# One expert of eight in split form: three reduced-precision products in place of full-precision matrix products, in an attention and mixture-of-experts kernel

## The chip, the cores and the metric

The kernel runs on one core of one Trainium2 chip. A core has engines that run side by side, each through its own list of instructions in order, and that wait for each other through semaphores: TensorE (PE, matrix products, its weight loads shown apart as PEld), VectorE (DVE), ScalarE (ACT), GpSimd (POOL) and SyncE (SP, which starts transfers). The metric is the device time of one execution, in microseconds (us); lower is better.

## What is computed

Three layers follow each other, in float32. Only the second and the third matter here.

```python
# layer 1: attention over a window and block summaries, x is 1536 tokens x 512
# layer 2: every token goes to one of E = 8 experts, cap = 192 tokens each
order = np.argsort(-flat)              # greedy: best logits first, experts fill up
...
for e in range(E):
    mask = assigned == e
    h = np.maximum(x[mask] @ w1[e], 0.0)      # 192x512 @ 512x1024
    out[mask] = h @ w2[e]                     # 192x1024 @ 1024x512
# layer 3: dense, on all tokens
h = x @ w_in                                  # 512 -> 1024
sm = e / (np.sum(e, axis=-1, keepdims=True) + 1e-09)   # e = exp(h - max)
solu = h * sm
ln = (solu - mu) / np.sqrt(var + 1e-06) * g_ln
return ln @ w_out                             # 1024 -> 512
```

## The kernel before

The attention runs first. Then come eight rounds, `for r in range(E)`, one expert each, in the order in which experts fill. A round multiplies its 192 tokens by w1 (`hidden`, 8 column blocks `f` by 4 blocks `c` of the depth) and by w2 (`product`, 4 blocks `d` by 8 blocks `c`): 32 and 32 matmuls with 128x128 weights and 192 moving columns, in plain float32. The profile shows each such matmul as two records, so 64 and 64 per round. The dense layer takes tiles of 128 tokens: one after an even round, two after an odd one (12 in all). `dense_in(n)` is the product with w_in and `dense_out(n)` that with w_out. These two are already in split form: each operand is a high part rounded to the type fp32r and a rest (`yT_hi`, `yT_lo`, `win_hi`, `win_lo`, ...), and three products hi*hi, hi*lo, lo*hi are added up in PSUM, 512 columns each. After round r = 6 comes tile 9 (`dense_in(9)`, `dense_out(8)`, in the middle of which the tokens of round 7 are transposed), after round r = 7 tiles 10 and 11.

What goes from PE to the other engines for reuse passes through two PSUM banks, `turn[u % 2]`, as numbered units u: PE fills one and raises `unit_filled`, ACT copies it to SBUF and raises `unit_emptied`, and `unit_free(u)` makes PE wait until unit u - 2 is emptied. A unit of `hidden` or `product` holds two blocks of 192 columns. For `product`, ACT writes `yT_hi` and DVE then writes the rest, `yT_lo` (`split_y`).

Every engine's order is written out by hand. Around the last expert ACT does, for round 6: the relus of `hidden`, the two copies of `yT_hi`, then for tile 9 `empty_turned(8)`, `hidden_exp(9)`, `empty_tokens(7)`, `empty_out(8)`, `hidden_squares(9)`; then the relus of round 7. DVE does `split_y(6, 0)`, `split_y(6, 1)`, `hidden_max(9)`, `split_turned(8)`, `hidden_gate(9)`, `hidden_spread(9)` (which needs the squares), then `split_y(7, 0)`. Weights come by indirect transfers that POOL starts (`gather_w1`, `gather_w2`) into the half `r % 2` of `w1_sb` and `w2_sb`, as soon as the expert two rounds earlier has been multiplied.

Of the kernel before, what the change touches and what calls it, by code (L numbers as in the profile page):

```python
# [5 lines left out]
ALU = mybir.AluOpType  # L6
ACT = mybir.ActivationFunctionType
AX = mybir.AxisListType
# [5 lines left out]
P = 128  # L14
# [49 lines left out]
ROUNDS = E - 1  # L64
PAIRS = E // 2
ROWS = PAIRS * TILES
MASK = -1e9
# [66 lines left out]


def unit_order():
    turned = 2
    for r in range(E):
        yield ("tokens", r), 2
        yield ("hidden", r), FC // 2  # L140
# [17 lines left out]
def build(nc, qT, kT, k_win, vT, v_main, v_tail, w_gate, w1, w2, w_in, w_out, g_ln, consts, digits, x_dram, out):  # L158
    with ExitStack() as ctx:
# [47 lines left out]
        vmean = sb("vmean", [P, D])  # L207

        key_wide = sb("key_wide", [P, NT * P])
        keys = sb("keys", [P, N])  # L210
        neg = keys[:, 0:4 * COLS].rearrange("p (s h c) -> p s h c", s=2, h=2)
# [5 lines left out]
        rden = sb("rden", [P, 2, 2])  # L217
        probT = key_wide[:, 0:6 * P].rearrange("p (s a c) -> p s a c", s=2, a=3)
        xs = sb("xs", [P, LOOP_UN, P])
        wg_sb = sb("wg_sb", [P, 2 * KC, E])  # L220
        xTg = key_wide[:, 6 * P:(6 + GATED) * P].rearrange("p (a c) -> p a c", a=GATED)
# [40 lines left out]


        w1_sb = sb("w1_sb", [P, 2, KC * FF])
        w2_sb = sb("w2_sb", [P, 2, FC * DM])

        kwin = [w[:, 1, 0:QT * SCOLS].rearrange("p (t c) -> p t c", t=QT) for w in (w1_sb, w2_sb)]
# [101 lines left out]
        in_x = [[sem(f"in_x{i}_{part}") for part in ("hi", "lo")] for i in range(2)]  # L369
        h_filled = sem("h_filled")  # L370
        hneg_ready = sem("hneg_ready")
        expo_ready = sem("expo_ready")
# [23 lines left out]
        at = unit_table()  # L396
        y_filled = [at["y", r, 1] + 1 for r in range(E)]
        turned_at = [at["norm", n] + 2 for n in range(ROWS)]
        y_unit = {at["y", r, d]: KC // 2 * r + d + 1 for r in range(E) for d in range(KC // 2)}
        norm_unit = {at["norm", n] + c: 2 * n + c + 1 for n in range(ROWS) for c in range(2)}  # L400

# [314 lines left out]
        def _(act):  # L716
# [72 lines left out]
            def empty_tokens(r):  # L789
# [4 lines left out]
                empty(u, xT[:, :, lo:lo + LO], turn[u % 2][:, 0:KC * LO].rearrange("p (c n) -> p c n", c=KC))  # L794

            def empty_hidden(r, f):
# [37 lines left out]
            for r in range(E):  # L834
                for f in range(FC // 2):
                    empty_hidden(r, f)
                for d in range(KC // 2):
                    empty_y(r, d)
                    if r != 1 and turns_keys(r, 2 * d + 1):
                        empty_keys(r + 2)  # L840
                if r == 1:
                    empty_keys(3, range(2))
                    hidden_exp(0)
                    empty_keys(3, range(2, KEY_UNITS))
                if r == 0:
                    empty_tokens(1)
                for n in tiles_after(r):
                    if n >= 1:
                        empty_turned(n - 1)
                        if n == 1:  # L850
                            hidden_squares(0)
                        hidden_exp(n)
                    if r and n == tiles_after(r)[-1] and r + 1 < E:
                        empty_tokens(r + 1)
# [10 lines left out]
        def _(pe):  # L865
# [127 lines left out]
            def unit_free(u):  # L993
                if u >= 2:
                    pe.wait_ge(unit_emptied, u - 1)
                if u - 2 in y_unit:
                    pe.wait_ge(y_lo_ready, y_unit[u - 2])
                if u - 2 in norm_unit:
                    pe.wait_ge(turned_lo_ready, norm_unit[u - 2])
# [69 lines left out]
            def product(r, d):  # L1069
# [14 lines left out]
                if d % 2:  # L1084
                    mm.then_inc(unit_filled, 1)

            def turn_unit(n, c):

# [9 lines left out]
            def dense_in(n):  # L1098
# [4 lines left out]
                for half in range(2):  # L1103
# [19 lines left out]
                    if half == 0 and j < 2:  # L1123
                        pe.wait_ge(y_lo_ready, 2 * (r + 1))
                    for c in range(KC):
# [39 lines left out]
            def rows_of_round(r):  # L1165
                if r < ROUNDS:
                    row_numbers(r)

            def warm(count):

# [19 lines left out]
            for r in range(E):  # L1190
# [20 lines left out]
                product(r, 3)  # L1211
                if r == 1:
# [29 lines left out]
        def _(dve):  # L1242
# [264 lines left out]
            def split_y(r, d):  # L1507
# [6 lines left out]
                                  yT_hi[part_of].bitcast(F32), ALU.subtract).then_inc(y_lo_ready, 1)  # L1514

            def split_turned(n):
                for c in range(2):
# [155 lines left out]
            for r in (E - 2, E - 1):  # L1673
                split_y(r, 0)
                split_y(r, 1)
                for n in tiles_after(r):
                    hidden_max(n)
                    split_turned(n - 1)
                    hidden_gate(n)
                    hidden_spread(n)  # L1680
            split_turned(ROWS - 1)
            link(dve.tensor_scalar(key_wide[:, N // 2:N].bitcast(BF16), hits, 0.5, 0.0, ALU.is_ge, ALU.add,
                                   accum_out=count[:, :]))
            link(dve.tensor_scalar(hits, keys[:, :], const("cand0"), None, ALU.is_ge))

# [88 lines left out]
```

## Time and profile before

| | |
|---|---|
| median of 3 runs | 498.69 us (498.5 to 498.85) |
| the profiled execution: its own time | 498.7 us |
| its span, first to last instruction | 496.9 us |
| busy: PE, DVE, ACT, POOL | 475.6, 343.5, 169.3, 137.4 us |
| mean granted TensorE clock | 0.993 |

The profiled execution is 1.8 us longer than its span (what lies around it). A time such as 435.24 below is in us from the span's start. Records of matmuls overlap: the time that one takes on the path is the distance from start to start, not its duration.

### The profile page before, as it was taken

The numbers are of one execution on the slowest core, as the hardware profiler recorded it, in microseconds if no ns is written. First come the engines' busy times: TensorE is split into PE (matmuls) and PEld (weight loads), VectorE is DVE, ScalarE is ACT, GpSimd is POOL, SyncE is SP. The second block draws the span as 40 slices with busy tenths as digits, with TensorE's granted clock in tenths as the row PEclk, the third lists the DMA queues.
The fourth block names the chain that finished last, engine by engine and source line by source line (L and its number), as shares of the span: only waits on it lengthen the run. The fifth ranks groups of instructions, "written<-read, shape, count | busy, mean of one in ns | idle before, by whom it ended". The sixth has DMA issues, their size and how long they took to land.

```text
span 496.9 us, 8519 instructions
## 1 busy us (share of the span) xinstructions
PE 475.6 (96%) x2907; PEld 412.5 (83%) x2907; DVE 343.5 (69%) x1180; ACT 169.3 (34%) x436; POOL 137.4 (28%) x206
## 2 busy tenths in 40 slices
PE   7999999989989999999999999999999999999992
PEld 4777777778779889788989988998997899899871
DVE  5777777569889898999869779986975610400451
ACT  3778888830021211343213123322312330320340
POOL 5886667520130130061131014113103231010101
PEclk9999999999999999999999999999999999999997
DMA  8877774110081460064243046034204528000001
GB/s 268 309 248 248 239 237 141 33 34 1 5 325 41 153 218 1 2 222 170 104 173 139 0 170 221 14 126 171 107 0 192 200 87 307 0 22 1 0 22 42
DMA packets 24920, 62.02 MB, mean 125 GB/s; under 512 B 6576, under 2 KB 13616, under 8 KB 20784
## 3 DMA queue, kind: packets, MB, share of 16 engines
q0 software_dynamic: 6592, 39.85, 22.0%
q1 hardware_dynamic: 17280, 20.44, 12.6%
q10 hardware_dynamic: 1008, 1.22, 0.8%
q8 instruction: 23, 0.38, 0.3%
q14 instruction: 17, 0.14, 0.1%
HBM read 55.21 MB, written 6.29 MB: 124 GB/s over the span
## 4 chain that ended last, share of the span: by engine, by line
PE 79%; DVE 13%; DMA 2%; issue 2%; ACT 1%; SPq 1%; POOL 0%; ACTq 0%; DVEq 0%; POOLq 0%
PE psum L1065 15%; PE psum L1082 13%; PE psum L883 6%; DVE key_wide L1406 5%; PE psum L1147 5%; PE psum L1154 5%; PE psum L1148 4%; PE psum L1116 4%; PE psum L1117 4%; PE psum L1126 4%; PE psum L912 4%; PE psum L892 3%; PE psum L909 2%; PE psum L1094 2%; DMA shared<-kT 2%
## 5 line engine op out<-in xcount | busy, mean ns | idle before, releaser
L1406 DVE TENSOR_SCALAR_CACHE_REDUCE key_wide<-keys,thr 128x1536 bf16<-128x1536 f32 x49 | 88.7, 1809 | 1.1
L1082 PE MATMUL psum<-xs,w_sb 128*128 128x192 f32 x512 | 87.0, 328 | 0.0
L1065 PE MATMUL psum<-shared,w_sb 128*128 128x192 f32 x512 | 84.6, 326 | 0.0
L1065 PEld LDWEIGHTS psum<-shared,w_sb 128*128 128x128 f32 x512 | 83.5, 190 | 1.1 <-issue 0.6
L1082 PEld LDWEIGHTS psum<-xs,w_sb 128*128 128x128 f32 x512 | 83.0, 190 | 0.0
L656 POOL DMA_INDIRECT w_sb<-w,widx x32 | 31.3, 979 | 95.4 <-DVE widx L1486 87.6
L680 POOL TENSOR_TENSOR gain<-spread,cst 128x1 f32<-128x1 f32 x12 | 6.8, 567 | 163.3 <-DVE spread L1546 163.3
L1285 DVE CUSTOM_DVE_ANT_0 keys<-psum,w_sb 128x184 f32<-128x184 f32 x96 | 29.7, 347 | 22.6 <-PE psum L883 14.2
L883 PE MATMUL psum<-w_sb,shared 128*128 128x376 f32 x96 | 43.1, 534 | 1.9 <-POOL w_sb L545 1.7
L1513 DVE TENSOR_TENSOR yT_lo<-psum,yT_hi 128x384 fp32r<-128x384 f32 x16 | 8.8, 554 | 51.7 <-ACT yT_hi L779 51.4
L741 ACT ACTIVATE keys<-keys,nmax 128x184 f32<-128x184 f32 x96 | 42.0, 440 | 7.0 <-DVE nmax L1285 6.9
L1147 PE MATMUL psum<-wout_hi,turned_hi 128*128 128x512 f32 x96 | 38.5, 401 | 0.7 <-ACT turned_hi L779 0.7
L1116 PE MATMUL psum<-win_hi,yT_hi 128*128 128x512 f32 x96 | 38.5, 401 | 0.0
L1148 PE MATMUL psum<-wout_lo,turned_hi 128*128 128x512 f32 x96 | 37.6, 391 | 0.0
L1117 PE MATMUL psum<-win_lo,yT_hi 128*128 128x512 f32 x96 | 37.5, 391 | 0.0
L779 ACT ACTIVATE xs<-psum 128x384 f32<-128x384 f32 x32 | 15.6, 489 | 59.0 <-PE psum L1065 59.0
L779 ACT ACTIVATE yT_hi<-psum 128x384 fp32r<-128x384 f32 x16 | 7.9, 491 | 79.5 <-PE psum L1082 79.5
L1172 PE MATMUL psum<-cst 128*128 128x256 f32 x150 | 34.5, 382 | 0.0
L892 PEld LDWEIGHTS psum<-cst,keys 128*128 128x128 f32 x144 | 19.1, 144 | 14.6 <-issue 8.8
L1172 PEld LDWEIGHTS psum<-cst 128*128 128x128 f32 x150 | 27.7, 189 | 3.8
L779 ACT ACTIVATE turned_hi<-psum 128x512 fp32r<-128x512 f32 x24 | 14.1, 597 | 48.2 <-PE psum L1094 48.2
L1126 PE MATMUL psum<-win_hi,yT_lo 128*128 128x512 f32 x96 | 28.6, 402 | 0.0
(176 smaller groups left out, 839.8 us busy)
## 6 DMA issues: line engine op xcount, KB each, us to landing
shared<-vT SPq DMA_DIRECT2D x8, 384.0 KB, 6.0
shared<-v_main SPq DMA_DIRECT2D x8, 384.0 KB, 3.1
x_rows<-xs SPq DMA_DIRECT2D x8, 384.0 KB, 4.8
shared<-kT SPq DMA_DIRECT2D x7, 384.0 KB, 5.5
shared<-qT SPq DMA_DIRECT2D x7, 384.0 KB, 4.9
w_sb<-w_in SPq DMA_DIRECT2D x4, 512.0 KB, 5.4
w_sb<-w_out SPq DMA_DIRECT2D x8, 256.0 KB, 4.6
shared<-v_tail SPq DMA_DIRECT2D x16, 48.0 KB, 3.1
```

What stands on the lines that cost most here:

```text
L741: act.activation(prob[:, s, HEAD1 * hh:HEAD1 * hh + COLS], neg[:, s, hh, :], ACT.Exp, bias=nmax[:, s, hh:hh + 1], scale=-1.0, accum_out=de ...
L779: return act.activation(dst, src, func).then_inc(unit_emptied, 1)
L883: pe.matmul(score[s][:, 0:SCOLS], q_sb[:, b, t * P:(t + 1) * P], kwin[b][:, t, :], start=True, stop=True).then_inc(scores_ready, 1)
L1065: mm = pe.matmul(turn[u % 2][:, i * CAP:(i + 1) * CAP], w1_sb[:, par, first:first + P], xT[:, c, :], start=(c == 0), stop=(c == KC - 1))
L1082: mm = pe.matmul(turn[u % 2][:, (d % 2) * CAP:(d % 2 + 1) * CAP], w2_sb[:, par, first:first + P], hT[:, c, :], start=(c == 0), stop=(c == ...
L1116: pe.matmul(out_cols, yT_hi[:, c, tile], win_hi[:, c, cols], start=(c == 0), stop=False)
L1117: pe.matmul(out_cols, yT_hi[:, c, tile], win_lo[:, c, cols], start=False, stop=False)
L1126: mm = pe.matmul(out_cols, yT_lo[:, c, tile], win_hi[:, c, cols], start=False, stop=(c == KC - 1))
L1147: pe.matmul(pv[:, :], turned_hi[:, c, :], wout_hi[:, c, :], start=(c == 0), stop=False)
L1148: pe.matmul(pv[:, :], turned_hi[:, c, :], wout_lo[:, c, :], start=False, stop=False)
L1172: pe.matmul(pv[:, 0:2 * P], ones_f, slots_f, start=True, stop=True)
L1406: link(dve.tensor_scalar(hits, keys[:, :], cand, -float(CAP), ALU.is_ge, ALU.add, accum_out=count[:, :]))
```

## The change

The last expert, r = 7, is computed in split form. `w1` and `w2` of that expert are rounded by ACT to high parts (four pieces of 128x1024 each), and DVE subtracts these from the raw weights for the rests, in place. The halves of `w1_sb` and `w2_sb` that expert 6 leaves free take the high parts (`w1_split`, `w2_split` lie at the same addresses), so the rounding of w1 waits for the end of `hidden` of round 6, and that of w2 for the end of its `product`. The tokens and the hidden values are kept as pairs (high, rest) side by side, 384 columns. PE multiplies the high weights by the pair (384 columns) and the rest of the weights by the high operand (192 columns), into two halves of a bank; so a unit is now one block `f` or `d`. DVE adds the two halves up (`add_pair`), ACT rounds the sum (relu or copy), and DVE writes the rest. Two DVE instructions at the very end, whose outputs nobody reads, are gone.

```diff
+SPLIT = (E - 1,)
+PIECES = 4
...
+            def round_w2(r, pieces):
+                act.wait_ge(in_w2[r % 2], 32 * (r // 2 + 1))
+                act.wait_ge(unit_filled, y_filled[r - 1])
+                for j in pieces:
+                    act.activation(w2_split[:, 1 - r % 2, piece(j)], w2_sb[:, r % 2, piece(j)],
+                                   ACT.Copy).then_inc(w2_hi_ready, 1)
...
             for r in range(E):
-                for f in range(FC // 2):
-                    empty_hidden(r, f)
-                for d in range(KC // 2):
-                    empty_y(r, d)
...
+                if r in SPLIT:
+                    for f in range(FC):
+                        empty_split_hidden(r, f)
+                    for d in range(KC):
+                        empty_split_y(r, d)
+                else:
+                    for f in range(FC // 2):
+                        empty_hidden(r, f)
+                    if r + 1 in SPLIT:
+                        round_w1(r + 1, range(PIECES))
...
+                    if r + 1 in SPLIT:
+                        round_w2(r + 1, range(2))
...
                     if 1 <= n < ROWS - 1:
                         hidden_squares(n)
+                if r + 1 in SPLIT:
+                    round_w2(r + 1, range(2, PIECES))
...
+            def split_products(u, high, low, pair, first, last):
+
+                both = turn[u % 2][:, 0:2 * CAP]
+                if not last:
+                    pe.matmul(both, high, pair.rearrange("p s n -> p (s n)"), start=first, stop=False)
+                mm = pe.matmul(turn[u % 2][:, 0:CAP], low, pair[:, 0, :], start=False, stop=False)
+                if last:
+                    mm = pe.matmul(both, high, pair.rearrange("p s n -> p (s n)"), start=False, stop=True)
+                return mm
...
                     if half == 0 and j < 2:
-                        pe.wait_ge(unit_emptied, at["y", r, 0] + 1)
+                        pe.wait_ge(unit_emptied, at["y", r, y_units(r) // 2 - 1] + 1)
                     for c in range(KC):
                         if half == 0 and j < 2 and c == KC // 2:
-                            pe.wait_ge(unit_emptied, at["y", r, 1] + 1)
+                            pe.wait_ge(unit_emptied, at["y", r, y_units(r) - 1] + 1)
...
+            def split_w2(r, pieces):
+                k = SPLIT.index(r)
+                for j in pieces:
+                    dve.wait_ge(w2_hi_ready, PIECES * k + j + 1)
+                    dve.tensor_tensor(w2_split[:, r % 2, piece(j)], w2_sb[:, r % 2, piece(j)],
+                                      w2_split[:, 1 - r % 2, piece(j)].bitcast(F32), ALU.subtract).then_inc(w2_lo_ready, 1)
+
+            def add_pair(u, k):
+
+                dve.wait_ge(unit_filled, u + 1)
+                dve.tensor_reduce(pair_sum[:, k % 2, :], turn[u % 2][:, 0:2 * CAP].rearrange("p (s n) -> p n s", s=2),
+                                  AX.X, ALU.add).then_inc(sum_ready, 1)
...
                 for n in tiles_after(r):
                     hidden_max(n)
                     split_turned(n - 1)
                     hidden_gate(n)
+                    if r + 1 in SPLIT:
+                        split_x(r + 1)
                     hidden_spread(n)
+                if r + 1 in SPLIT:
+                    split_w2(r + 1, range(2, PIECES))
```

This is ACT's order from the exponentials of tile 9 (L816) on, before: the tokens' two copies, the output of tile 8 (L829), the squares of tile 9 (L821), and then the four relus of round 7 into `xs`.

```order
L816 ACTIVATE shared,hsum<-psum,hneg 128x1024
L779 ACTIVATE shared<-psum 128x4x128
L779 ACTIVATE shared<-psum 128x4x64
L829 ACTIVATE shared<-psum,gain 128x512
L821 ACTIVATE shared,squares<-shared 128x1024
L779 ACTIVATE xs<-psum 128x384 x4
L779 ACTIVATE yT_hi<-psum 128x2x192 x2
```

The same stretch of ACT's order in the changed kernel (`w_split` is the weights' high parts, `pair_sum` the sums that DVE makes, `h_low` and `h_high` the hidden values of blocks 0 to 3 and 4 to 7):

```order
L892 ACTIVATE shared,hsum<-psum,hneg 128x1024
L823 ACTIVATE x_pair<-psum 128x4x128
L823 ACTIVATE x_pair<-psum 128x4x64
L905 ACTIVATE shared<-psum,gain 128x512
L897 ACTIVATE shared,squares<-shared 128x1024
L869 ACTIVATE w_split<-w_sb 128x1024 x2
L849 ACTIVATE h_low<-pair_sum 128x192 x4
L849 ACTIVATE h_high<-pair_sum 128x192 x4
L855 ACTIVATE yT_hi<-pair_sum 128x192 x4
```

Two roundings of 128x1024 now stand between the squares and the first relu, and there are eight relus in place of four.

On DVE, before, the gate of tile 9 (last instruction L1539) and its spread (L1546) are followed straight by the rests of round 7's output:

```order
L1539 TENSOR_SCALAR shared<-shared,gmean 128x1024
L1546 SCALAR_TENSOR_TENSOR spread<-squares,hfloor 128x1
L1513 TENSOR_TENSOR yT_lo<-psum,yT_hi 128x2x192 x2
L1526 TENSOR_REDUCE hneg<-psum 128x1
```

DVE's order at the same place in the changed kernel, up to the second block's sum and beyond:

```order
L1742 TENSOR_SCALAR shared<-shared,gmean 128x1024
L1664 TENSOR_TENSOR x_pair<-psum,x_pair 128x4x128
L1664 TENSOR_TENSOR x_pair<-psum,x_pair 128x4x64
L1749 SCALAR_TENSOR_TENSOR spread<-squares,hfloor 128x1
L1679 TENSOR_TENSOR w_split<-w_sb,w_split 128x1024 x2
L1685 TENSOR_REDUCE pair_sum<-psum 128x192 x2
L1690 SCALAR_TENSOR_TENSOR h_low<-pair_sum,h_low 128x192
L1685 TENSOR_REDUCE pair_sum<-psum 128x192
L1690 SCALAR_TENSOR_TENSOR h_low<-pair_sum,h_low 128x192
```

The tokens' rests stand ahead of the spread, and two subtractions of 128x1024 stand between the spread and the first sum of round 7.

## Rows read from the trace of the kernel before

**Rows 1.** The page: granted TensorE clock in 40 slices, in tenths.

```profile
PEclk9999999999999999999999999999999999999997
```

**Rows 2.** Chain that ended last, in order of time: start us, us, what.

```profile
435.40 10.40 PE psum L1065 x64
...
485.33 1.83 PE psum L1154 x8
```

**Rows 3.** Timeline of PE, last part: start us, us, instruction.

```profile
435.24 10.56 PE L1065 MATMUL psum<-shared,w_sb 128*128 128x192 f32 x64
...
455.90 0.53 PE L1116 MATMUL psum<-win_hi,yT_hi 128*128 128x512 f32 x1
456.26 0.40 PE L1117 MATMUL psum<-win_lo,yT_hi 128*128 128x512 f32 x1
...
478.10 1.98 PE L1154 MATMUL psum<-wout_hi,turned_lo 128*128 128x512 f32 x8
479.92 1.03 PE L1094 MATMUL psum<-cst,shared 128*128 128x128 f32 x8
481.44 0.47 PE L1147 MATMUL psum<-wout_hi,turned_hi 128*128 128x512 f32 x1 [0.48 <-ACT turned_hi L779]
```

**Rows 4.** Timeline of PE in the attention: matmuls of 8 columns.

```profile
101.88 0.79 PE L948 MATMUL psum<-wg_sb,key_wide 128*128 128x8 f32 x6
102.53 0.47 PE L909 MATMUL psum<-shared,key_wide 120*128 120x128 f32 x2
```

**Rows 5.** Timeline of ACT around the last expert.

```profile
417.22 0.49 ACT L779 ACTIVATE yT_hi<-psum 128x384 fp32r<-128x384 f32 x1 [4.71 <-PE psum L1082]
...
427.87 0.60 ACT L779 ACTIVATE turned_hi<-psum 128x512 fp32r<-128x512 f32 x1 [4.96 <-PE psum L1094]
...
433.00 0.87 ACT L779 ACTIVATE shared<-psum 128x512 f32<-128x512 f32 x2 [2.19 <-PE psum L1050]
...
436.02 1.05 ACT L821 ACTIVATE shared<-shared 128x1024 f32<-128x1024 f32 x1
436.96 0.19 ACT L821 ACTIVATION_READ_ACCUMULATOR shared<-shared 128x1 f32 x1
438.03 0.49 ACT L779 ACTIVATE xs<-psum 128x384 f32<-128x384 f32 x1 [0.88 <-PE psum L1065]
...
480.70 1.08 ACT L779 ACTIVATE turned_hi<-psum 128x512 fp32r<-128x512 f32 x2
```

**Rows 6.** Line L779 on ACT by shape: duration ns min/median/max.

```profile
L779 ACT ACTIVATE yT_hi<-psum x4: 490/491/492, 417.2 to 456.2; 128x384 fp32r<-128x384 f32 x4
L779 ACT ACTIVATE shared<-psum x3: 379/379/598, 399.7 to 433.5; 128x256 f32<-128x256 f32 x2, 128x512 f32<-128x512 f32 x1
```

**Rows 7.** Timeline of DVE around the last expert.

```profile
428.35 1.22 DVE L1526 TENSOR_REDUCE hneg<-psum 128x1 f32<-128x1024 f32 x1 [4.84 <-PE psum L1126]
...
431.28 1.22 DVE L1535 SCALAR_TENSOR_TENSOR shared<-psum,shared 128x1024 f32<-128x1024 f32 x1
...
432.73 0.75 DVE L1539 TENSOR_SCALAR shared<-shared,gmean 128x1024 f32<-128x1024 f32 x1
...
451.56 0.56 DVE L1513 TENSOR_TENSOR yT_lo<-psum,yT_hi 128x384 fp32r<-128x384 f32 x1 [14.21 <-ACT yT_hi L779]
...
485.91 1.02 DVE L1684 TENSOR_SCALAR key_wide<-keys,cst 128x1536 bf16<-128x1536 f32 x1
```

**Rows 8.** DMA of line L656 issued at 407.1: the second half of w1 for round 7.

```profile
L656 POOL DMA_INDIRECT w_sb<-w,widx x1: 962/962/962, 407.1 to 407.1; - x1
...
DMA to landing us min/median/max: 7.6/7.6/7.6
```

**Rows 9.** Windows at the end: us, PE, PEld, DVE, ACT, POOL busy, PEclk, DMA share, GB/s.

```profile
489.00:490.00 1.00, 0.00 (x0) 0.00 (x0) 0.00 (x0) 0.00 (x0) 0.64 (x1) 1.00 0.00 0
490.00:491.00 1.00, 0.00 (x0) 0.00 (x0) 0.00 (x0) 0.00 (x0) 0.00 (x0) 0.61 0.69 262
491.00:492.00 1.00, 0.00 (x0) 0.00 (x0) 0.00 (x0) 0.00 (x0) 0.00 (x0) 0.50 0.00 0
```

More of the change, by code:

```diff
@@ L133, in turns_keys, with hidden_units, y_units, y_before @@
     return r + 2 < ROUNDS and d == (1 if r % 2 == 0 and r else 3)
+def hidden_units(r):
+    return FC if r in SPLIT else FC // 2
+def y_units(r):
+    return KC if r in SPLIT else KC // 2
+def y_before(r):
+    return sum(y_units(i) for i in range(r))
 def unit_order():
@@ L139, in unit_order @@
         yield ("tokens", r), 2
-        yield ("hidden", r), FC // 2
-        for d in range(KC // 2):
+        yield ("hidden", r), hidden_units(r)
+        for d in range(y_units(r)):
             yield ("y", r, d), 1
@@ L396, in build, with piece @@
         at = unit_table()
-        y_filled = [at["y", r, 1] + 1 for r in range(E)]
+        y_filled = [at["y", r, y_units(r) - 1] + 1 for r in range(E)]
         turned_at = [at["norm", n] + 2 for n in range(ROWS)]
-        y_unit = {at["y", r, d]: KC // 2 * r + d + 1 for r in range(E) for d in range(KC // 2)}
+        y_unit = {at["y", r, d]: y_before(r) + d + 1 for r in range(E) for d in range(y_units(r)) if r not in SPLIT}
+        x_unit = {at["tokens", r] + i: 2 * k + i + 1 for k, r in enumerate(SPLIT) for i in range(2)}
+        SUMS = FC + KC
+        def piece(j):
+            return slice(j * KC * FF // PIECES, (j + 1) * KC * FF // PIECES)
         norm_unit = {at["norm", n] + c: 2 * n + c + 1 for n in range(ROWS) for c in range(2)}
@@ L1211, in _, with warm @@
                 product(r, 3)
+            def warm(count):
+                for i in range(count):
+                    pe.matmul(pv[:, 0:2 * P], ones_f, slots_f, start=True, stop=True)
+            pe.wait_ge(consts_ready, 1)
+            warm(WARM_TURN)
+            turn_keys(0)
+            warm(WARM_SEARCH)
+            cuts(0)
+            warm(WARM_RANKS)
+            member_ranks(0)
+            warm(WARM_ROWS)
+            row_numbers(0)
+            warm(WARM_KEYS)
+            turn_keys(1)
+            pe.wait_ge(win_lo_ready, 2 * KC)
+            pe.wait_ge(wout_lo_ready, 2 * FC)
+            warm(WARM_TOKENS)
+            tokens(0)
+            warm(1)
+            for r in range(E):
+                if r in SPLIT:
+                    for f in range(FC):
+                        hidden_split(r, f)
+                    for d in range(KC):
+                        product_split(r, d)
+                else:
+                    products(r)
                 if r == 1:
@@ L1514, in split_y, with split_x @@
                                   yT_hi[part_of].bitcast(F32), ALU.subtract).then_inc(y_lo_ready, 1)
+            def split_x(r):
+                k = SPLIT.index(r)
+                for i, (first, n) in enumerate(zip(slots_of(r), (HI, LO))):
+                    u = at["tokens", r] + i
+                    dve.wait_ge(unit_emptied, u + 1)
+                    dve.tensor_tensor(x_pair[:, :, 1, first:first + n],
+                                      turn[u % 2][:, 0:KC * n].rearrange("p (c n) -> p c n", c=KC),
+                                      x_pair[:, :, 0, first:first + n].bitcast(F32), ALU.subtract).then_inc(x_lo_ready, 1)
@@ new lines, in split_pair_y, with split_expert @@
+            def split_pair_y(r, d):
+                first = (r % 2) * CAP
+                dve.wait_ge(unit_emptied, at["y", r, d] + 1)
+                dve.tensor_tensor(yT_lo[:, d, first:first + CAP], pair_sum[:, d % 2, :],
+                                  yT_hi[:, d, first:first + CAP].bitcast(F32), ALU.subtract).then_inc(y_lo_ready, 1)
+            def split_expert(r):
+                k = SPLIT.index(r)
+                for f in range(FC):
+                    if f >= 2:
+                        dve.wait_ge(h_lo_ready, FC * k + f - 1)
+                    add_pair(at["hidden", r] + f, f)
+                    if f:
+                        split_hidden(r, f - 1)
+                split_hidden(r, FC - 1)
+                for d in range(KC):
+                    if d < 2:
+                        dve.wait_ge(h_lo_ready, FC * (k + 1) - 1 + d)
+                    else:
+                        dve.wait_ge(y_lo_ready, y_before(r) + d - 1)
+                    add_pair(at["y", r, d], d)
+                    if d:
+                        split_pair_y(r, d - 1)
+                split_pair_y(r, KC - 1)
```

126 lines of the change are left out of this document (96 added, 30 removed).

## The prediction

> **What bounds the kernel now.** I read the page first, then the chain that ended last, then the timelines of PE, ACT and DVE around the last expert. The chain runs on PE through the whole stage: the first product of round 7 stands in it as one piece of 10.40 us for 64 records [rows 2], the second as another of the same size, and the timeline shows no idle time ahead of either [rows 3]. PE works at the full clock throughout [rows 1]. So here a nanosecond saved on PE is one saved, and one in which PE waits is lost. ACT and DVE are far from full in this stage: DVE's next work after the tile's gate and spread is the rest of round 7's output, at 451.56 [rows 7], and ACT does a relu of 0.49 us every 2.6 us. What matters is when they get to the work that PE needs back.
>
> **PE's own work.** A plain float32 matmul of 192 columns is two records of 10.40 / 64 = 162.5 ns, so 325 ns, and 64 of them make 20.80 us. In their place come 64 pairs in fp32r, one of 384 columns and one of 192. No fp32r matmul of such a size is in this trace; those of 512 columns follow each other in (479.92 - 478.10) / 8 = 227.5 ns [rows 3], 0.444 ns a column. By that, 384 columns take 171 ns; with the excess over 512 columns at 2.4 GHz put as a fixed part (14 ns) they take 174. I take 173. The 192 columns would stream in 85 ns, but every matmul needs its own weights: six of only 8 columns follow each other in (102.53 - 101.88) / 6 = 108 ns [rows 4], so a load of 128x128 weights costs about that, hidden only behind a longer stream. I take 110. A pair is 283 ns, 64 pairs are 18.1 us: **2.7 us less**. Bounds of a pair: 256 ns (171 + 85, no load showing), and 498 ns (173 + 325, if the short one ran at the float32 pace).
>
> **The wait that it brings.** PE starts round 7 at 435.24 [rows 3] and can fill two units before it needs one back. A unit is now 4 pairs, 1.13 us, so both are full at 437.50. The first comes back after DVE's sum and ACT's relu, and each of them has two weight pieces of 128x1024 in its queue ahead of that. ACT: the squares and their read-out end at 436.96 + 0.19 = 437.15 [rows 5]; a piece costs as much as the squares, 1.05 us for the same size, so the pieces end at 438.20 and 439.25. DVE: each piece needs ACT's; a two-input operation on 128x1024 takes 1.22 us [rows 7], I take 1.2, so 438.23 to 439.43 and on to 440.63. Only now comes the first sum: 384 elements from PSUM, 0.56 as in L1513 [rows 7], to 441.19. The relu of 192 columns: ACT's copies take 379 ns for 256 and 491 for 384 [rows 6], so 0.32 for 192; with 0.03 to start, 441.54. From ACT to PE 0.14 us, as in the last tile (first copy ends at 480.70 + 0.60 = 481.30 [rows 5], PE starts at 481.44 [rows 3]). PE goes on at 441.68: **4.2 us idle**. If DVE's piece took only the 0.75 us of the one-input L1539 [rows 7], ACT's pace would bind and the wait be 0.6 us shorter.
>
> **The loop of two banks.** From filled to free again a unit now takes 0.19 (relu at 438.03 [rows 5], the unit's 16 records streamed until 435.24 + 2.60 = 437.84) + 0.56 + 0.03 + 0.32 + 0.14 = 1.24 us, against 1.13 for filling the other. So of the six remaining hidden units every second one waits 0.11 us, as does the first output unit: **0.3 us**. Output units have 8 pairs, 2.26 us, and don't wait.
>
> **The end of the round.** `dense_in(10)` needs the last output block after four matmuls, that is 0.36 us for the first (455.90 to 456.26 [rows 3]) and 3 x 0.2275, together 1.04. Before, the copy of 0.49 us was back in time. Now it takes 1.24: **0.2 us**.
>
> **What I cost at nothing.** The rounding of w1: its last half lands 7.6 us after 407.06 [rows 8], at 414.7; four ACT pieces then last until 418.9 and delay the copy of round 6's first output, due at 417.22 [rows 5], by 1.7 us, but PE needs that only in the dense tile about 5 us after it was due. DVE ends at about 420.6, before the second copy (about 422.4) and before the rests are wanted. The first two pieces of w2 lie between that copy and ACT's next work at 427.87 [rows 5]; DVE is through them at about 426.4, next due at 428.35 [rows 7]. Without that cover each piece would cost 1.0 to 1.2 us. The tokens' rests: ACT is done at 433.87 [rows 5], and DVE's two operations (some 0.7 and 0.4 us, the first beside ACT's second copy) end near 434.6, before 435.24. The two DVE instructions dropped at the end finish at 486.93 [rows 7], inside PE's last matmuls, to 487.16 [rows 2]: nothing.
>
> **Sum.** -2.7 + 4.2 + 0.3 + 0.2 = +2.0 us. The profiled execution took 498.7 us, the median of the runs is 498.69, so 500.7 us. About 0.2%, 1.0 us, is what a measurement of this kernel can tell from no change.
>
> **Rivals.**
>
> *The clock falls in the wait.* At the end of the program PE stopped at 487.16 [rows 2] and the granted clock, 1.00 until 490.00, had a mean of 0.61 in the next us and was 0.50 after it [rows 9]: it fell about 3.1 us after the last matmul. That is from 2.4 to 1.2 GHz. My wait of 4.2 us is longer. Against it: it is one fall, barely shorter than my wait. If the clock takes as long to rise again once PE works (an estimate from the same 3.1 us), half of 3.1 us of work is lost, 1.6 us: 502.3, and twice that at most, 503.8. The Trainium skill, "TensorE: Matmul & The Clock Gate", section "What's actually happening", says that the slow clock is the default and that activity releases it; by that rule, the trace agrees, 502.3 is to be expected rather than 500.7 once the wait is long enough.
>
> *The pair costs only its stream.* With 256 ns and no load showing, the product of 32 pairs saves 0.9 us more, the six hidden units, held by the 1.24 us of the banks, only 0.3: 499.5, and with DVE's piece at 0.75 us 498.9. This is no change. Against it stand the 108 ns of [rows 4]. The same page, section "Back-to-back issue gap", has columns / 2.4 GHz + 2.5 ns, 162.5 + 82.5 = 245 ns a pair, by which it would be about 499.2; the rows of 512 columns (227.5 ns, where the rule has 215.8) don't bear it out.
>
> *The short matmul runs at the float32 pace,* 325 ns in place of 110. Nothing in the trace speaks for it but that no fp32r matmul below 512 columns is there. Outside the wait stand 56 pairs: 56 x 0.215 = 12.0, less 0.3 for the banks: 512.4.
>
> *Faster: the roundings don't hold PE up.* DVE and ACT have more than 10 us of free time in the stage before. If the last two pieces of w2 were through by 437.5, the 4.2 us would go and -2.1 remain: 496.6. The point from which it decides is the first sum: the kernel is faster by over 0.2% only if PE idles less than 4.2 - 2.0 - 1.0 = 1.2 us, so if the sum begins before about 437.6. Against it stand two ACT pieces that can't begin before 437.15 and are in the queue ahead of the relu.
>
> **How the numbers follow.** Clock stays, as summed: 0.56. Clock falls: 0.23. Short matmul dear: 0.08. Cheap pair: 0.08. Faster: 0.05. The predicted time is that of the first. From 499.2 (cheap pair) to 503.9 (the clock's upper bound) the range leaves out the dear matmul and the faster case, and little at the edges. Faster 0.05; within 0.2% 0.09, the cheap pair and a sliver of the first case; slower 0.86.
>
> **What would show it.** PE's timeline should have its first matmul of round 7 at about 435.2, idle time of about 4 us after the second hidden unit, ended by ACT's relu, and a start of `dense_in(10)` about 1.9 us later than before. DVE should do its two pieces of w2 from 438.2 to 440.6. A mean granted clock clearly below 0.993, or 0.50 in a window behind the wait, is the second case. I am wrong if PE doesn't idle there, or if pairs follow each other in much other than 283 ns; 256 ns would show in the output product, where nothing waits.

## The result: 502.4 us, the split expert is 0.8% slower

| | before | changed |
|---|---|---|
| median | 498.60 us (498.26 to 498.85, 4 runs) | 502.41 us (502.28 to 503.15, 4 runs) |
| span of the profiled execution | 496.9 us | 500.5 us |
| mean granted TensorE clock | 0.993 | 0.986 |
| from round 7's first matmul to the span's end | 496.9 - 435.24 = 61.7 us | 500.5 - 434.72 = 65.8 us |

The ratio is 1.0081, 95% interval [1.0063, 1.0098]. The time lies inside the stated range, but it is that of the second case of the prediction (the clock falls in the wait, 502.3 us, given a chance of 0.23), not of the likeliest (500.7). The last line of the table is the one by which the experiments below are read too: everything ahead of round 7 varies by a microsecond or two between executions (here it was 0.5 us shorter), and the last line leaves that out.

Only half of what the mean granted clock lost belongs to the change. In the profile of the changed kernel the clock fell twice while PE had work left: behind the new wait, which the windows below show, and at 104.4 us in the attention, where nothing was changed. Each time it was down for 3.4 us, which takes 0.0034 off the mean.

The timeline of PE in the changed kernel, of the first two hidden units, the wait, and the units after it (L1184 and L1187 are matmuls with high weights, L1185 those with the weights' rest):

```profile
434.72 0.34 PE L1184 MATMUL psum<-x_pair,w_split 128*128 128x384 f32 x1
...
436.82 0.36 PE L1187 MATMUL psum<-x_pair,w_split 128*128 128x384 f32 x1
440.90 0.44 PE L1184 MATMUL psum<-x_pair,w_split 128*128 128x384 f32 x1 [3.72 <-ACT h_low L849]
...
442.49 0.57 PE L1184 MATMUL psum<-x_pair,w_split 128*128 128x384 f32 x1
...
443.02 0.57 PE L1184 MATMUL psum<-x_pair,w_split 128*128 128x384 f32 x1
443.39 0.57 PE L1185 MATMUL psum<-x_pair,w_split 128*128 128x192 f32 x2
...
452.25 0.33 PE L1184 MATMUL psum<-h_low,w_split 128*128 128x384 f32 x1
452.43 0.25 PE L1185 MATMUL psum<-h_low,w_split 128*128 128x192 f32 x1
...
454.56 0.34 PE L1184 MATMUL psum<-h_low,w_split 128*128 128x384 f32 x1
...
459.16 0.39 PE L1248 MATMUL psum<-win_hi,yT_hi 128*128 128x512 f32 x1
```

Two things are to be seen. PE sat idle for 3.72 us until ACT's relu, where [rows 3] has none. And behind that the same matmuls take longer: 0.57 us in place of 0.36. The windows say why (us, PE, PEld, DVE, ACT and POOL busy, granted clock, DMA share, GB/s):

```profile
437.00:440.80 3.80, 0.18 (x1) 0.00 (x0) 3.18 (x4) 1.85 (x3) 2.56 (x2) 1.00 0.13 49
440.80:442.00 1.20, 1.10 (x8) 1.10 (x9) 0.44 (x2) 0.41 (x2) 0.00 (x0) 1.00 0.22 79
442.00:443.00 1.00, 1.00 (x7) 1.00 (x6) 0.58 (x2) 0.00 (x0) 0.00 (x0) 0.66 0.00 0
443.00:445.00 2.00, 2.00 (x10) 2.00 (x9) 0.80 (x3) 0.36 (x1) 0.00 (x0) 0.50 0.00 0
445.00:446.00 1.00, 1.00 (x6) 1.00 (x6) 0.27 (x2) 0.36 (x1) 0.00 (x0) 0.64 0.00 0
446.00:449.00 3.00, 3.00 (x20) 2.78 (x20) 1.81 (x5) 0.73 (x2) 0.00 (x0) 1.00 0.00 0
```

The clock was still at 1.00 during the whole wait. It fell to 0.50 (1.2 of 2.4 GHz) at about 442.3, 1.4 us after PE had started again, and was back at 445.7. (The moments are worked out from the mean of the window in which the clock changes: a mean of 0.66 is 0.32 us at 1.00 and 0.68 us at 0.50.) The chain that ended last shows what PE waited for, each step released by the one above it:

```profile
434.94 0.56 issue
435.50 1.14 ACT shared L897 x2
436.64 0.96 ACT w_split L869
437.62 2.36 DVE w_split L1679 x2
439.98 0.48 DVE pair_sum L1685
440.48 0.37 ACT h_low L849
440.90 0.44 PE psum L1184
```

These are the squares of tile 9, one ACT rounding, DVE's two subtractions, the sum and the relu, in the order that the prediction has. The first of them starts when PE has just begun round 7.

### The profile page after: what moved, and what is told of

It is laid out like the page before. It is cut to its first block, busy times and chain, and to the rows that moved or that the text cites. A ratio compares the mean times of both kernels' runs of the same rounds, so it can differ in the third digit from the quotient of the medians.

```text
span 500.5 us, 8578 instructions
## 1 busy us (share of the span) xinstructions
PE 475.1 (95%) x2907; PEld 411.1 (82%) x2907; DVE 359.9 (72%) x1209; ACT 178.0 (36%) x450; POOL 138.4 (28%) x206
## 4 chain that ended last, share of the span: by engine, by line
PE 78%; DVE 14%; issue 2%; DMA 2%; ACT 2%; SPq 1%; POOL 0%; ACTq 0%; DVEq 0%; POOLq 0%
PE psum L1158 12%; PE psum L1175 11%; PE psum L974 6%; DVE key_wide L1548 5%; PE psum L1279 5%; PE psum L1286 5%; PE psum L1280 4%; PE psum L1248 4%; PE psum L1249 4%; PE psum L1258 4%; PE psum L1003 4%; PE psum L983 3%; PE psum L1000 2%; PE psum L1184 2%; PE psum L1226 2%
## 5 line engine op out<-in xcount | busy, mean ns | idle before, releaser
L1175 PE MATMUL psum<-xs,w_sb 128*128 128x192 f32 x448 | 76.4, 328 | 0.0
L1158 PE MATMUL psum<-shared,w_sb 128*128 128x192 f32 x448 | 74.1, 326 | 0.0
L1158 PEld LDWEIGHTS psum<-shared,w_sb 128*128 128x128 f32 x448 | 73.0, 190 | 1.0 <-issue 0.6
L1175 PEld LDWEIGHTS psum<-xs,w_sb 128*128 128x128 f32 x448 | 72.6, 190 | 0.0
L974 PE MATMUL psum<-w_sb,shared 128*128 128x376 f32 x96 | 40.8, 507 | 2.4 <-POOL w_sb L589 1.8
L1328 PE MATMUL psum<-cst 128*128 128x256 f32 x150 | 35.9, 393 | 0.0
L823 ACT ACTIVATE xs<-psum 128x384 f32<-128x384 f32 x28 | 13.7, 489 | 51.8 <-PE psum L1158 51.8
L823 ACT ACTIVATE yT_hi<-psum 128x384 fp32r<-128x384 f32 x14 | 6.8, 489 | 64.1 <-PE psum L1175 64.1
L793 ACT ACTIVATE key_wide<-psum 128x384 f32<-128x384 f32 x48 | 23.2, 484 | 11.7 <-PE psum L983 11.4
```

Source lines behind the costliest of these rows:

```text
L823: return act.activation(dst, src, func).then_inc(unit_emptied, 1)
L974: pe.matmul(score[s][:, 0:SCOLS], q_sb[:, b, t * P:(t + 1) * P], kwin[b][:, t, :], start=True, stop=True).then_inc(scores_ready, 1)
L1158: mm = pe.matmul(turn[u % 2][:, i * CAP:(i + 1) * CAP], w1_sb[:, par, first:first + P], xT[:, c, :], start=(c == 0), stop=(c == KC - 1))
L1175: mm = pe.matmul(turn[u % 2][:, (d % 2) * CAP:(d % 2 + 1) * CAP], w2_sb[:, par, first:first + P], hT[:, c, :], start=(c == 0), stop=(c == ...
L1328: pe.matmul(pv[:, 0:2 * P], ones_f, slots_f, start=True, stop=True)
```

## The experiments

All times "from round 7 on" are span minus start of the first split matmul in the profiled execution. Each kernel was timed beside runs of the kernel before on the same chip; these scatter more than above (some 497 to 501.5 us), so the ratios have wider intervals.

**Idle matmuls in the wait.**

```diff
                     for f in range(FC):
                         hidden_split(r, f)
+                        if f == 1:
+                            for i in range(8):
+                                pe.matmul(small[:, 0:2 * P], ones_f, slots_f, start=True, stop=True)
```

> The changed kernel with eight plain float32 matmuls of 256 columns on constants, into a spare bank, put behind the second hidden unit of round 7, where PE otherwise idles; they add no work that anything waits for and take about 8 x 0.43 = 3.4 us of a wait of 3.9 us. Theory A (the wait costs 3.9 us, and the clock that falls after it another 1.5 to 1.6 us): the clock stays at 1.00, the third unit still starts when ACT's first relu is done, and the kernel takes 502.4 - 1.5 = 500.9 us. Rival B (the low clock in the records is no cost of its own, or comes from the split products themselves): 502.4 us, and the granted clock still falls in this stage.

Median 501.67 us against 498.7 for the kernel before, ratio 1.0059 [1.0038, 1.0081]. From round 7 on: 501.0 - 436.64 = 64.4 us, against 65.8. PE's timeline:

```profile
438.95 3.62 PE L1352 MATMUL psum<-cst 128*128 128x256 f32 x16
442.83 0.44 PE L1184 MATMUL psum<-x_pair,w_split 128*128 128x384 f32 x1 [0.26 <-ACT h_low L849]
```

The third unit starts 6.19 us after the first, as in the changed kernel (440.90 - 434.72 = 6.18), the clock is at 1.00 in all windows of this stretch, and 1.4 us are gone. So the fall of the clock is a cost of its own, of the size expected (1.5). The medians say less: 2.97 us above the kernel before in place of 3.81, and the intervals of the two ratios overlap. In this profile the part ahead of round 7 was 1.4 to 1.9 us longer, with two falls of the clock there (at 105.3 and 146.3 us); such falls blur the medians of all these kernels.

**All roundings early.**

```diff
-                        round_w2(r + 1, range(2))
+                        round_w2(r + 1, range(PIECES))
...
-                if r + 1 in SPLIT:
-                    round_w2(r + 1, range(2, PIECES))
...
-                        split_w2(r + 1, range(2))
+                        split_w2(r + 1, range(PIECES))
...
-                if r + 1 in SPLIT:
-                    split_w2(r + 1, range(2, PIECES))
```

> The changed kernel with the last two pieces of w2 rounded by ACT and split by DVE together with the first two, right after the output of round 6 is emptied, so that nothing stands ahead of the first sum and the first relu of round 7. Theory A: the wait of 3.9 us and the fall of the clock both go, PE's own saving of 2.3 us stays, less 0.3 us for the two banks and 0.2 to 0.3 us at the dense tile: about 498.6 - 1.7 = 496.9 us. Rival C (the roundings are only displaced: four pieces in a row make DVE late for the maximum of tile 9 and ACT late for its exponentials, and PE waits there instead): 499 us or more, with PE idle in tile 9's stage. Rival B (split products cost more than the float32 ones, the wait only shows it): still above 498.6 us.

Median 498.61 us, ratio 0.9999 [0.998, 1.0018]. From round 7 on: 495.8 - 434.56 = 61.24 us, against 61.66 before the change. The big wait and the fall of the clock are gone, and tile 9 is not late (round 7 starts 23.41 us after the start of round 6's output product, in the kernel before 23.42), so rival C is out; rival B is answered by the price of a pair, 289 ns below where the float32 matmuls take 325. But only 0.4 us is left of the saving, where 1.7 was expected. DVE's and ACT's timelines show where the rest went:

```profile
436.52 0.16 DVE L1747 SCALAR_TENSOR_TENSOR spread<-squares,hfloor 128x1 f32<-128x1 f32 x1 [2.54 <-ACT shared L897]
436.60 1.02 DVE L1683 TENSOR_REDUCE pair_sum<-psum 128x192 f32<-128x384 f32 x2
```

```profile
437.18 0.84 ACT L849 ACTIVATE h_low<-pair_sum 128x192 fp32r<-128x192 f32 x2 [0.69 <-DVE pair_sum L1683]
439.71 0.36 ACT L849 ACTIVATE h_low<-pair_sum 128x192 fp32r<-128x192 f32 x1 [1.69 <-DVE pair_sum L1683]
440.87 0.36 ACT L849 ACTIVATE h_low<-pair_sum 128x192 fp32r<-128x192 f32 x1 [0.79 <-DVE pair_sum L1683]
442.25 0.36 ACT L849 ACTIVATE h_high<-pair_sum 128x192 fp32r<-128x192 f32 x1 [1.02 <-DVE pair_sum L1683]
443.39 0.36 ACT L849 ACTIVATE h_high<-pair_sum 128x192 fp32r<-128x192 f32 x1 [0.78 <-DVE pair_sum L1683]
444.79 0.36 ACT L849 ACTIVATE h_high<-pair_sum 128x192 fp32r<-128x192 f32 x1 [1.03 <-DVE pair_sum L1683]
```

The first sum still stands behind the spread, and the spread behind the squares, so PE waits for the third unit:

```profile
437.60 0.45 PE L1182 MATMUL psum<-x_pair,w_split 128*128 128x384 f32 x1 [0.57 <-ACT h_low L849]
```

It starts 3.04 us after the first, where two units of four pairs take 2.31, so this costs 0.7 us. From then on relus follow each other by 1.16, 1.38, 1.14, 1.40 us: every second unit is 0.24 us late, where I had 0.11.

**One rounding late, twice, and with idle matmuls.** The edit is that of the early roundings with three pieces early (`range(3)`) and the fourth left behind the squares.

> The changed kernel with three pieces of w2 early and only the fourth left behind the squares. Theory A: one piece less is ahead of the first sum, 1.0 us on ACT and 1.2 us on DVE, so PE waits 3.9 - 1.2 = 2.7 us. If the clock stays up in a wait of that length, 502.4 - 1.2 - 1.5 = 499.7 us; if it falls as before, 501.2 us. A rival by which ACT, not DVE, sets the end of the wait (1.0 us a piece) gives 2.9 us of wait, so 0.2 us more in either case.

Median 502.55 us, ratio 1.0091 [1.0061, 1.0121]. In its profile PE idled 2.58 us before the third unit, the clock stayed at 1.00, and from round 7 on it took 499.1 - 435.85 = 63.3 us, which would make 500.3. The timed runs were well above that, with mean clocks from 0.988 down to 0.976. Those means don't say where the clock fell: the profiled execution has 0.988, and its fall was in the attention, from 105 to 112 us. So the kernel was run again, beside one with five idle matmuls (`range(5)` in the edit above) and the changed kernel itself.

> The kernel with one rounding left late once more. Its first profile had no fall of the clock in the wait of 2.6 us and took 63.25 us from the start of round 7, which would make 500.3 us, but its timed runs had a median of 502.55 and mean clocks from 0.988 down to 0.976. Theory F (the clock falls in this wait in some executions and not in others): mean clocks spread again below 0.985, and the median lies above that of the same kernel with the wait filled by idle matmuls. Rival (the runs were late for other reasons): the two have the same median.

> One rounding late, and five idle float32 matmuls of 256 columns (2.2 us) in the wait. Theory F: no fall of the clock here in any run, 63.25 us from the start of round 7, about 500.3 us, 1 to 2 us less than the same kernel without them. Rival: the same as without them.

> The changed kernel as it is, beside the next two on one chip, to see whether the clock falls in every one of its runs. Theory A (an idle stretch of 3.7 us brings it down each time): the granted clock is 0.50 for some 3 us behind the wait in this profile too, from the start of round 7 to the end it takes 65.8 us, the median is about 502.4 us. A rival by which the fall depends on where the wait happens to lie: in this profile no fall or a shorter one, 64.3 us.

One late again: median 501.38 us, ratio 1.0063 [1.0043, 1.0083]. This time the same wait (2.59 us) did bring the clock down:

```profile
441.00:442.00 1.00, 0.26 (x1) 0.26 (x2) 1.00 (x3) 0.57 (x2) 0.76 (x1) 1.00 0.00 0
442.00:443.00 1.00, 1.00 (x8) 1.00 (x8) 0.08 (x1) 0.15 (x1) 0.00 (x0) 0.96 0.68 258
443.00:444.00 1.00, 1.00 (x5) 1.00 (x5) 0.63 (x2) 0.04 (x1) 0.00 (x0) 0.50 0.08 21
...
446.00:447.00 1.00, 1.00 (x7) 1.00 (x7) 0.32 (x2) 0.36 (x1) 0.00 (x0) 0.84 0.00 0
```

It fell at about 442.9, 1.2 us after PE's restart at 441.74, and from round 7 on it took 501.3 - 436.69 = 64.6 us, 1.3 more than the other profile of the same kernel. With five idle matmuls: median 500.27 us, ratio 1.004 [1.0025, 1.0056], no fall, 498.4 - 435.09 = 63.3 us. That is the 500.3 expected, with ten runs between 499.7 and 501.2, against eight between 501.1 and 503.4 without them, on the same chip. The mean clocks of the eight spread less than expected, three at 0.983 and five from 0.988 to 0.990.

The changed kernel again: median 502.53 us, ratio 1.008 [1.0057, 1.0103]. Its wait is the same, 3.72 us, but here the clock fell inside it:

```profile
436.00:438.00 2.00, 0.55 (x4) 0.30 (x3) 1.17 (x2) 1.91 (x3) 1.49 (x2) 1.00 0.00 0
438.00:440.00 2.00, 0.00 (x0) 0.00 (x0) 2.00 (x4) 0.14 (x1) 1.16 (x1) 0.71 0.16 59
440.00:441.00 1.00, 0.73 (x3) 0.73 (x4) 0.61 (x2) 0.58 (x2) 0.00 (x0) 0.50 0.38 143
...
445.00:446.00 1.00, 1.00 (x7) 1.00 (x6) 0.82 (x2) 0.37 (x1) 0.00 (x0) 0.67 0.00 0
```

It was down from about 438.8 to 445.7, 5.4 us of that while PE worked, and from round 7 on it took 500.7 - 434.09 = 66.6 us, where 65.8 was expected. So the fall cost 1.4 us in one execution and, by the same difference to 64.4, 2.2 in another. Both fit the rows: at 0.50 a pair takes 0.53 us (443.02 - 442.49 above) in place of 0.289, so 3.4 us of work lose 1.55 us and 5.4 us lose 2.5, and in both one wait of 0.24 for the two banks would have been there anyway and is covered. That is an estimate of 1.3 and 2.2 us.

**The clock also falls where no wait is long.** In the attention of the changed kernel's first profile:

```profile
103.43 0.61 PE L1039 MATMUL psum<-wg_sb,key_wide 128*128 128x8 f32 x4 [0.47 <-ACT key_wide L801]
104.57 0.60 PE L1039 MATMUL psum<-wg_sb,key_wide 128*128 128x8 f32 x2 [0.37 <-ACT key_wide L801]
```

```profile
103.00:104.00 1.00, 0.57 (x5) 0.58 (x5) 0.96 (x10) 0.37 (x1) 0.00 (x0) 1.00 0.00 0
104.00:105.00 1.00, 0.63 (x4) 0.44 (x4) 0.07 (x1) 0.28 (x1) 0.00 (x0) 0.70 1.03 313
```

The waits are 0.47 and 0.37 us, with a few short matmuls between them, and the clock fell at 104.4. In the kernel before the same two waits are followed by one of 1.37 us, and the clock stayed at 1.00. In the profile of the kernel with eight idle matmuls it fell at 146.3, 1.5 us after PE had started again behind a wait of 1.54 us. So the length of the longest wait doesn't decide.

**What a pair costs.** With the early roundings, the short matmul narrowed to 64 of its 192 columns, and then left out; both leave out part of the products.

```diff
-                mm = pe.matmul(turn[u % 2][:, 0:CAP], low, pair[:, 0, :], start=False, stop=False)
+                mm = pe.matmul(turn[u % 2][:, 0:64], low, pair[:, 0, 0:64], start=False, stop=False)
```

> As the kernel with all roundings early, but the matmul of the weights' rest takes 64 of the 192 columns only; it leaves out two thirds of that partial product. It asks what sets the 289 ns of a pair. Theory L (the load of weights of the next matmul, about 108 ns, is what the short matmul has to cover): pairs stay at 280 to 289 ns, the time stays at about 496.9 us. Rival S (columns alone: a short matmul costs its stream): a pair falls by 128 x 0.444 = 57 ns to about 232 ns, which in the output product's 32 pairs is 1.8 us, and little in the hidden part, which the two banks hold: about 494.9 us.

> As the kernel with all roundings early, but without the matmul of the weights' rest; it leaves out that partial product. With 64 columns in place of 192 a pair still took 287 ns. Theory L (a load of weights, about 108 ns, has to be covered, and the short matmul doesn't cover it): with one weight load less the rest of the pair, a matmul of 384 columns, follows its like in 171 to 174 ns, an output unit of 8 in 1.4 us in place of 2.3. A rival by which a matmul of 384 columns needs more than its stream even alone (the starts from a long one to its short one lie 200 ns apart): 200 ns or more, 1.6 us a unit. The hidden units are held by the two banks in both.

Narrow: median 498.41 us, ratio 0.9996 [0.9976, 1.0016], from round 7 on 498.0 - 436.81 = 61.2 us, all as with 192 columns. Left out: 493.39 us, ratio 0.9892 [0.9866, 0.9918]. Two output units of the narrow kernel, and then one of the kernel without the short matmul:

```profile
449.83 0.33 PE L1182 MATMUL psum<-h_low,w_split 128*128 128x384 f32 x1
450.00 0.19 PE L1183 MATMUL psum<-h_low,w_split 128*128 128x64 f32 x1
...
452.12 0.33 PE L1182 MATMUL psum<-h_low,w_split 128*128 128x384 f32 x1
```

```profile
445.45 0.86 PE L1182 MATMUL psum<-h_low,w_split 128*128 128x384 f32 x4
446.14 0.68 PE L1182 MATMUL psum<-h_high,w_split 128*128 128x384 f32 x3
446.66 0.34 PE L1185 MATMUL psum<-h_high,w_split 128*128 128x384 f32 x1
446.83 0.85 PE L1182 MATMUL psum<-h_low,w_split 128*128 128x384 f32 x4
```

Between the starts of two output units lie (452.12 - 449.83) / 8 = 286 ns a pair with 64 columns, (454.56 - 452.25) / 8 = 289 with 192, and (446.83 - 445.45) / 8 = 173 for the 384 alone. 128 columns are worth 3 ns, the matmul as such 113. That is about what the load of weights costs by [rows 4], 108 ns. The Trainium skill, "TensorE: Matmul & The Clock Gate", section "LDWEIGHTS (loading the stationary operand)", gives the number of weight columns over 1.2 GHz, 107 ns here; the trace agrees for these weights of four bytes. A fixed price of any matmul it is not: in the kernel before, matmuls of 2 columns with new weights in bf16 (two bytes) follow each other in (172.79 - 171.95) / 24 = 35 ns.

```profile
171.95 0.91 PE L1038 MATMUL psum<-token_b,shared 128*128 128x2 bf16 x24
172.79 1.20 PE L1126 MATMUL psum<-win_hi,yT_lo 128*128 128x512 f32 x4
```

No run has a narrow fp32r matmul that keeps its weights, so that the load sets the 113 ns, and nothing else that comes with four-byte operands, is the likeliest reading and not shown.

**Four banks in place of two** for the hidden units of round 7, with the late roundings left as they are, and then with the early ones:

```diff
+        def bank_of(u):
+            f = u - at["hidden", E - 1]
+            return bank[f % 4 - 2] if f < FC and f % 4 >= 2 else turn[u % 2]
...
-                unit_free(u)
+                if f < 2:
+                    unit_free(u)
+                elif f >= 4:
+                    pe.wait_ge(unit_emptied, u - 3)
```

> The changed kernel with the late roundings left as they are, but the hidden units of round 7 go round four PSUM banks in place of two, so PE can fill four before it needs one back. Theory A: PE fills until about 4.6 us after the start of the round, the first relu is done 6.1 us after it, so PE idles 1.6 us in place of 3.9, the clock stays at 1.00, and the waits of the two banks go too: from the start of round 7 to the end of the span about 61.5 us against 65.8, some 498.1 to 498.6 us in all. Rival D (DVE's sums, 0.9 us a unit, then become the pace, or the clock falls in two shorter waits as well): over 500 us.

> Both: all roundings early and four banks for the hidden units. With early roundings alone PE still waited 0.7 us for the first unit (squares and spread of tile 9 are ahead of relu and sum) and 0.24 us at three more units. Theory A: these 1.5 us go and the saving of the split products shows: from the start of round 7 to the end about 61.24 - 1.5 = 59.7 us against 61.7 before the change, so about 2.0 us below the kernel before, ratio 0.996. Rival E (PE gains no more than early roundings alone because the wait only moves to the first output unit, whose hidden rests come late): 61.2 us, ratio 0.999.

Late: median 498.83 us, ratio 1.0006 [0.999, 1.0022]; PE idled 1.41 us in the hidden part, once, the clock stayed at 1.00 there, and from round 7 on it took 497.4 - 435.77 = 61.6 us.

```profile
441.95 0.44 PE L1188 MATMUL psum<-x_pair,w_split 128*128 128x384 f32 x1 [1.41 <-ACT h_low L853]
```

Early: median 496.9 us against 498.74, ratio 0.997 [0.9954, 0.9985]; no idle time on PE in the hidden part, and 494.6 - 434.63 = 60.0 us, where 59.7 was expected; most of the rest is the wait that the last experiment takes away. So either cure on its own takes the long wait and the fall away and brings the kernel back to the time before, and only both together show a gain.

**The dense tile behind the round.** As the last one, and `dense_in(10)` takes the first two depth blocks of both output halves before it waits for the last block.

```diff
+                if n == ROWS - 2:
...
+                    for c in range(KC):
+                        if c == KC // 2:
+                            pe.wait_ge(unit_emptied, at["y", r, y_units(r) - 1] + 1)
+                        if c % 2 == 0:
+                            for half in range(2):
+                                for k in (c, c + 1):
```

> As that, and the first dense tile after the round multiplies the first two depth blocks for both halves of its output before it needs the last output block of round 7: 8 matmuls, 1.8 us, in place of 4 against the 1.24 us that the block takes to come back. Theory A: the wait of 0.2 us at that place goes, the stretch is 0.2 to 0.3 us shorter than with four banks and early roundings alone. A rival by which that wait is only moved (to the rests of the output, DVE's last instruction of the round): no difference.

Median 496.8 us, ratio 0.9961 [0.9947, 0.9975]. From round 7 on: 495.4 - 435.92 = 59.5 us, 0.5 less than without it, and the idle time ahead of the fifth matmul of `dense_in(10)` is gone, which the kernel with four banks and early roundings still had:

```profile
454.57 0.50 PE L1253 MATMUL psum<-win_hi,yT_hi 128*128 128x512 f32 x1 [0.19 <-ACT yT_hi L859]
```

The medians of the two differ by 0.1 us, which these runs can't tell apart; the trace can. By the ratio this version is 0.4% faster than the kernel before.

## Why the prediction was right, and where it was off

**What binds, and the order of the wait: right.** PE idle behind the second hidden unit, ended by ACT's relu, with DVE's two subtractions ahead of the first sum, is what the chain shows, step by step.

**PE's own work: right, and for the stated reason.** I had 283 ns a pair, 173 + 110; it is 289, with 173 and 113 to 116 as its parts. 64 pairs save 20.80 - 18.5 = 2.3 us where I had 2.7. The rival "the pair costs only its stream" is refuted by the 64 columns that cost what 192 do, and "the short matmul runs at the float32 pace" by 289 ns. The rule that the prediction takes from the Trainium skill, "TensorE: Matmul & The Clock Gate", section "Back-to-back issue gap", gives 245 ns a pair and doesn't fit. The section itself says that the rule is for a matmul taken alone and leaves out the load of weights, so it was not a fair rival for these pairs.

**The wait: right within 0.3 us.** I had the third unit at 6.44 us after the first; it started after 6.18 (idle 3.9 us from the end of eight pairs of 289 ns, at 437.03, and 3.72 by the record's end). ACT's rounding began at 436.55, while the read-out of the squares was still in its record, and two pieces of ACT and of DVE took 1.99 and 2.36 us where I had 2.1 and 2.4.

**The loop of two banks: a term of the sum too small.** I had three waits of 0.11 us; with the roundings out of the way they are 0.24 each, 0.7 us in all. The way back of a unit is some 0.15 us longer than the 1.24 that I added up, and the waits don't shrink with it. The trace of the changed kernel holds most of it. The sum of the seventh unit starts 0.27 us after PE is through with it (448.57 to 448.84), where I had 0.19, the relu 0.59 later, and PE 0.42 after that (449.85), 1.28 in all; and the first matmul after a wait takes 0.08 us longer (0.44 against 0.36). Four banks removed all of it.

**The end of the round: a term too small.** I had 0.2 us; taking the wait away gave 0.5. I had let the four matmuls ahead of the wait cover 1.04 us, with 0.36 for the first as in [rows 3]. Here all four follow at the usual pace and cover 4 x 0.2275 = 0.91, the wait ends 1.28 us after the first (459.16 to 460.44), and the matmul behind it takes 0.33 in place of 0.23: 0.37 + 0.10 us.

```profile
460.44 0.50 PE L1248 MATMUL psum<-win_hi,yT_hi 128*128 128x512 f32 x1 [0.19 <-ACT yT_hi L855]
```

**The sum without the clock** is then -2.3 + 3.9 + 0.7 + 0.5 = +2.8 us, and the run with idle matmuls, from round 7 on, has 64.4 - 61.7 = +2.7, where I had +2.0.

**The clock: the step that failed.** I held against a fall that it was only one, 3.1 us after the last matmul and barely shorter than my wait, and gave it 0.23. Both profiles of the changed kernel show it, and so does one of two with a wait of only 2.6 us, shorter than that 3.1. What I had wrong is the picture of a clock that falls once an idle stretch has lasted long enough: in two of three profiles it fell 1.2 to 1.4 us after PE was at work again, and in the attention it fell behind waits under 0.5 us. What does decide it, and why the same code has a fall in one execution and none in another, these runs leave open. The sign that I named, a mean clock clearly below 0.993, is not one either: half of the drop came from the attention, and runs of the kernel before beside the experiments have means from 0.982 to 0.996. The windows behind the wait are the sign. The price of 1.6 us that I worked out was right in size (1.4, 1.3, and 2.2 us when it fell inside the wait). With it the sum is 2.7 + 1.4 = 4.1 us in the trace, and 502.4 us in the runs.

**How good the number is.** That 502.3, the time of the second case, meets 502.4 within 0.1 us is in part luck. Its terms without the clock were 0.8 us too low, the clock's 0.2 too high, and the stage ahead of round 7, where nothing was expected, came out 0.5 us shorter in the profile. The likeliest case, 500.7, was wrong, and the time lies in the range because the range took in the second.

**The faster rival** was right in its mechanism: it had 496.6 us for roundings that are through in time. Early roundings alone came to 498.6, because squares and spread of tile 9 were still ahead of the first sum and two banks too few; with four banks 496.9. The small terms close the account: 2.3 - 0.7 (third unit) - 0.7 (two banks) - 0.5 (end of the round) = 0.4 us, which is what early roundings gained from round 7 on.

**What I cost at nothing** was nothing: the early roundings of w1 and of half of w2, the tokens' rests, and in the experiment even all of w2 fit in beside tile 9.

## What to carry to other kernels

When operands have to be prepared on the engines that also empty PSUM, look at where that preparation stands in their queues: the matmuls saved 2.3 us, and two weight pieces in the wrong place cost 3.9 and a fall of the clock. A wait on PE of two and a half microseconds or more had two prices here, its length and, in three of four profiles, one or two microseconds of lost time at the slow clock; more PSUM banks, or idle matmuls where nothing else helps, saved the second. Don't take that length for a threshold, and don't read such a fall off a mean clock: look at the windows around the wait. A short fp32r matmul with weights of its own cost about 115 ns here with 64 columns as with 192, so the columns between came free. And compare two kernels from the start of the changed stage: falls of the clock elsewhere move the whole time by a microsecond or two.

## What the runs showed of the hardware

- fp32r matmuls of 384 columns with new weights each follow each other in 173 ns, those of 512 in 227.5 [rows 3]. A short one between them adds 113 to 116 ns, with 64 columns or with 192. bf16 matmuls of 2 columns with new weights follow in 35 ns.
- In round 7 the clock fell at waits of 3.72 us (two profiles of two) and 2.6 us (one of two), not at those of 1.41 and 1.47 us (four banks with late roundings; the short matmul left out) or 0.57 us. It fell 1.4 and 1.2 us after PE's restart in two cases, and once 1.4 us ahead of it; the moments are worked out from the mean clock of the window in which it changed.
- In the attention it fell at 104.4 us behind waits of 0.47 and 0.37 us among short matmuls in one profile of the changed kernel, and not in that of the kernel before, with the same waits and one of 1.37 us.
- It was down for 3.4 us in the first two falls of round 7, for 3.4 us in that of the attention, and for 6.8 us in the third of round 7. A pair of 384 and 192 columns takes 0.53 us at the low clock and 0.289 us at the high one.
